# Reordering of inverse sums, weight units and first slot in a fused attention and two-layer kernel

## What is computed

```python
scores = cap * np.tanh(scale * np.matmul(q, k.transpose(0, 1, 3, 2)) / cap)
attn = np.exp(scores - np.max(scores, axis=-1, keepdims=True))
attn = attn / (np.sum(attn, axis=-1, keepdims=True) + 1e-09)
x = np.matmul(attn, v)                      # heads side by side: 896 x 768
h = x @ w_in                                # 768 -> 2048
x = np.where(h > 0.0, h, np.exp(np.minimum(h, 0.0)) - 1.0) @ w_out
h = x @ w_in2
return np.maximum(0.01 * h, h) @ w_out2
```

## Time and profile before

| | us |
|---|---|
| median of 3 runs (574.10 to 576.91) | 575.11 |
| the profiled execution's own time | 574.71 |
| its span | 572.9 |

### The profile page before, as it was taken

One profiled execution on the slowest core, in us unless ns is written; L12 is line 12 of the kernel. 1 busy time (PEld: TensorE's weight loads), 2 busy tenths in 40 slices (PEclk: granted clock), 3 DMA queues, 4 the chain that ended last, 5 costly groups with the idle time before them and its releaser, 6 DMA issues.

```text
span 572.9 us, 8610 instructions
## 1 busy us (share of the span) xinstructions
PE 556.7 (97%) x2908; PEld 499.4 (87%) x2908; DVE 469.4 (82%) x758; ACT 352.8 (62%) x606; POOL 275.2 (48%) x273
## 2 busy tenths in 40 slices
PE   6999989999999999999999999989999999999997
PEld 5777779889998999999999999879999998999997
DVE  5899998878875133898988999889999779999881
ACT  6999988999995455654644454536454445544440
POOL 6779998799965655552000003856666530000000
DMA  6455564455423333335644332031113225536251
GB/s 174 106 143 128 150 174 125 123 130 146 98 65 89 98 112 110 111 108 165 213 135 158 131 99 67 1 110 56 57 55 90 77 84 192 159 119 220 84 170 51
DMA packets 34172, 67.07 MB, mean 117 GB/s; under 512 B 6864, under 2 KB 18768, under 8 KB 34128
## 3 DMA queue, kind: packets, MB, share of 16 engines
q1 hardware_dynamic: 33984, 66.28, 39.4%
q10 hardware_dynamic: 144, 0.23, 0.1%
HBM read 63.70 MB, written 2.80 MB: 116 GB/s over the span
## 4 chain that ended last, share of the span: by engine, by line
PE 77%; DVE 10%; ACT 4%; issue 3%; POOL 3%; DMA 2%; ACTq 0%; SPq 0%; DVEq 0%; POOLq 0%
PE mlp_ps L1129 8%; PE mlp_ps L1131 8%; PE mlp_ps L1130 8%; PE o_ps L1129 6%; PE o_ps L1131 6%; PE o_ps L1130 6%; PE scores L1129 4%; PE scores L1130 4%; PE scores L1131 4%; PE probs_t L1103 4%; PE probs_t L1131 4%; PE probs_t L1130 4%; PE probs_t L1129 4%; PE scores L1088 2%; PE o_ps L1122 2%
## 5 line engine op out<-in xcount | busy, mean ns | idle before, releaser
L559 POOL TENSOR_TENSOR w_lo<-w_raw,w_hi 128x768 fp32r<-128x768 f32 (+1 forms) x62 | 104.2, 1681 | 62.3 <-ACT w_hi L621 61.9
L559 POOL TENSOR_TENSOR w_lo<-s_sum,w_hi 128x384 fp32r<-128x384 f32 x32 | 38.8, 1228 | 114.5 <-ACT w_hi L621 114.5
L621 ACT ACTIVATE w_hi<-s_sum 128x768 fp32r<-128x768 f32 (+1 forms) x64 | 43.4, 684 | 76.6 <-DVE s_sum L880 51.9
L621 ACT ACTIVATE w_hi<-w_raw 128x768 fp32r<-128x768 f32 (+1 forms) x77 | 56.5, 737 | 31.1 <-PE o_ps L1131 15.7
L601 ACT ACTIVATE soft<-soft,neg_max 112x448 f32<-112x448 f32 x96 | 63.6, 673 | 1.8 <-DVE soft L758 1.7
L758 DVE TENSOR_SCALAR_CACHE_REDUCE soft<-soft,neg_abs 112x448 f32<-112x448 f32 x96 | 60.9, 671 | 2.2 <-ACT soft L591 1.9
L1129 PE MATMUL mlp_ps<-x_hi,w_hi 128*128 128x448 f32 x132 | 49.2, 373 | 0.4 <-issue 0.4
L765 DVE TENSOR_TENSOR p_lo<-probs_t,p_hi 112x896 fp32r<-112x896 f32 x37 | 40.3, 1089 | 10.0 <-ACT p_hi L610 9.9
L1130 PE MATMUL mlp_ps<-x_lo,w_hi 128*128 128x448 f32 x132 | 48.2, 365 | 0.0
L1131 PE MATMUL mlp_ps<-x_hi,w_lo 128*128 128x448 f32 x132 | 48.2, 365 | 0.0
L591 ACT ACTIVATE soft<-scores 112x896 f32<-112x896 f32 x47 | 43.4, 924 | 6.0 <-PE scores L1089 5.9
(11 more groups left out here) (238 smaller groups left out, 1747.7 us busy)
## 6 DMA issues: line engine op xcount, KB each, us to landing
w_raw<-w_units SPq DMA_DIRECT2D x120, 384.0 KB, 3.2
q_raw<-qT SPq DMA_DIRECT2D x24, 224.0 KB, 3.1
k_raw<-kT SPq DMA_DIRECT2D x23, 224.0 KB, 3.0
v_raw<-v_rows SPq DMA_DIRECT2D x24, 112.0 KB, 3.2
inv_all<-inv_rows SPq DMA_DIRECT2D x24, 112.0 KB, 3.4
y_t<-y_out SPq DMA_DIRECT2D x12, 224.0 KB, 2.8
inv_rows<-row_inv SPq DMA_DIRECT2D x24, 1.8 KB, 3.1
k_raw<-kT ACTq DMA_DIRECT2D x1, 224.0 KB, 3.1
```

Source lines behind the costliest of these rows:

```text
L559: pool.tensor_tensor(w_part(w_lo, n), w_source(n), f32(w_part(w_hi, n)), ALU.subtract).then_inc(w_lo_pool, 1)
L621: nc.scalar.activation(w_part(w_hi, n), w_source(n), ACT.Copy).then_inc(w_hi_done, 1)
```

## The change

- SyncE: `store_inv` goes to the head of the odd step 2h+3, `load_inv` to the end of the even step 2h+4, behind the loads of k and q; loads of units go ahead of v.
- VectorE: `scale_o` goes from step 2h+7 to 2h+6, `w_high` of the first three units one step ahead. GpSimd: `x_parts` of the first four pairs go two steps ahead.
- Tables: step 30 has one chunk instead of three, step 54 ten instead of eight; a unit's last chunk is placed behind four chunks of the next unit, so that units end in every second step from 31 on.
- First slot: tanh and maxima tile by tile, the scale read from its column, the split of k of head 1 behind the maxima. All exponentials: each waits for its own tile's maximum.
- Border: the third `x_sum` comes ahead of a `weight_sum`, the last `weight_sum` of block 1 behind `y21`; in the first blocks the sums of (0, p6) and (0, p3) come ahead of `x_low("p2")`, and `block_hidden(0, "p3")` ahead of the sum of (0, p7).

```diff
@@ -2,2 +2,4 @@
+import itertools
+
 import numpy as np
@@ -47,3 +49,3 @@
 EARLY = {24: ((0, (0, 1, 2)),), 25: ((0, (3,)),), 26: ((1, (0, 1, 2)),), 27: ((1, (3,)),), 28: ((2, (0, 1, 2)),),
-         29: ((2, (3,)),), 30: ((0, (4,)), (1, (4,)), (2, (4,)))}
+         29: ((2, (3,)),), 30: ((0, (4,)),)}
@@ -56,3 +58,3 @@
          **{s: (1, 1, 0) for s in range(35, 48, 2)}, 48: (2, 1, 0), 49: (1, 2, 0), 50: (2, 1, 0), 51: (2, 0, 4),
-         52: (0, 0, 6), 53: (0, 0, 6), 54: (0, 0, 8)}
+         52: (0, 0, 6), 53: (0, 0, 6), 54: (0, 0, 10)}
@@ -64,3 +66,4 @@
-LATER = [(0, 5), (1, 5), (3, 0), (3, 1), (2, 5)] + [(u, c) for u in range(3, MAT_UNITS) for c in range(KC) if u > 3 or c > 1]
+LATER = [(0, 5), (1, 4), (1, 5), (3, 0), (2, 4), (3, 1), (3, 2), (3, 3), (2, 5), (3, 4)] + [
+    chunk for u in range(4, MAT_UNITS) for chunk in [(u, c) for c in range(4)] + [(u - 1, 5), (u, 4)]] + [(MAT_UNITS - 1, 5)]
@@ -74,6 +77,4 @@
     for n in MIXED.get(s, (0, 0, 0)):
-        place = {}
-        for u, c in LATER[done:done + n]:
-            place.setdefault(u, []).append(c)
-        places.append(list(place.items()))
+        runs = itertools.groupby(LATER[done:done + n], lambda chunk: chunk[0])
+        places.append([(u, [c for _, c in run]) for u, run in runs])
         done += n
@@ -162,3 +163,3 @@
 def x_step(m):
-    return 4 * m + (9 if 2 * m >= DIRECT else 11)
+    return 4 * m + 9
@@ -298,2 +299,3 @@
         y_stored = sem("y_stored")
+        first_scores, first_tanh = sem("first_scores"), sem("first_tanh")
         zero_set, ident_set, ident_ready = sem("zero_set"), sem("ident_set"), sem("ident_ready")
@@ -485,2 +487,9 @@
                     load_w(u + AHEAD + RAW)
+
+                if s % 2 == 1 and 0 <= (s - 3) // 2 < NHEAD:
+                    store_inv((s - 3) // 2)
+                if s in FIRST_LOADS:
+                    load_w(FIRST_LOADS.index(s))
+                if s % 2 == 1 and 2 <= s // 2 + 1 < NHEAD:
+                    load_v(s // 2 + 1)
                 if s % 2 == 0 and s // 2 + 4 < NHEAD:
@@ -488,10 +497,4 @@
                     load_q(s // 2 + 4)
-                if s % 2 == 1 and 0 <= (s - 5) // 2 < NHEAD:
-                    load_inv((s - 5) // 2)
-                if s % 2 == 1 and 2 <= s // 2 + 1 < NHEAD:
-                    load_v(s // 2 + 1)
                 if s % 2 == 0 and 0 <= (s - 4) // 2 < NHEAD:
-                    store_inv((s - 4) // 2)
-                if s in FIRST_LOADS:
-                    load_w(FIRST_LOADS.index(s))
+                    load_inv((s - 4) // 2)
             for r in range(units_ending_at(STEPS - 1)[0] + AHEAD + RAW, len(RAW_ROWS)):
@@ -587,2 +590,11 @@
             def tanh(k):
+                if k == 0:
+
+                    act.wait_ge(first_scores, 1)
+                    nc.scalar.activation(soft[0:QT, 0, 0, :], scores[0:QT, 0, 0:SEQ], ACT.Tanh, scale=s_scale[0:QT, 0:1]
+                                         ).then_inc(first_tanh, 1)
+                    act.wait_ge(scores_done, 1)
+                    nc.scalar.activation(soft[0:QT, 0, 1, :], scores[0:QT, 1, 0:SEQ], ACT.Tanh, scale=s_scale[0:QT, 0:1]
+                                         ).then_inc(tanh_done, 1)
+                    return
                 act.wait_ge(scores_done, k + 1)
@@ -596,3 +608,2 @@
                 b, c = k % SOFT, k % 2
-                act.wait_ge(neg_max_done, 2 * k + 2)
                 if half == 0 and h >= 2:
@@ -600,2 +611,3 @@
                 for t in range(2):
+                    act.wait_ge(neg_max_done, 2 * k + t + 1)
                     nc.scalar.activation(soft[0:QT, b, t, :], soft[0:QT, b, t, :], ACT.Exp, bias=neg_max[:, c, t:t + 1],
@@ -696,4 +708,5 @@
             act.wait_ge(cap_ready, 1)
-            act.reg_load(scale_reg, s_scale[0:1, 0:1].bitcast(mybir.dt.int32))
             for s in range(STEPS):
+                if s == 1:
+                    act.reg_load(scale_reg, s_scale[0:1, 0:1].bitcast(mybir.dt.int32))
                 if s < SLOTS:
@@ -755,4 +768,7 @@
                 b, c = k % SOFT, k % 2
-                dve.wait_ge(tanh_done, k + 1)
+                if k:
+                    dve.wait_ge(tanh_done, k + 1)
                 for t in range(2):
+                    if k == 0:
+                        dve.wait_ge(*((first_tanh, 1), (tanh_done, 1))[t])
                     nc.vector.tensor_scalar(soft[0:QT, b, t, :], soft[0:QT, b, t, :], neg_abs[0:QT, 0:1], BIG, ALU.mult,
@@ -981,3 +997,2 @@
             nc.vector.tensor_scalar(s_scale[:, :], cap_inv[:, :], float(HD) ** -0.5, None, ALU.mult).then_inc(cap_ready, 1)
-            split_k0(1)
             for s in range(STEPS):
@@ -985,2 +1000,4 @@
                     maxima(s)
+                if s == 0:
+                    split_k0(1)
                 for u in units_ending_at(s - 1):
@@ -991,6 +1008,6 @@
                     invert((s - 3) // 2)
-                if s in (12, 16, 20):
-                    w_high((s - 12) // 4)
-                if s % 2 == 1 and 0 <= (s - 7) // 2 < DIRECT:
-                    scale_o((s - 7) // 2)
+                if s in (11, 15, 19):
+                    w_high((s - 11) // 4)
+                if s % 2 == 0 and 0 <= (s - 6) // 2 < DIRECT:
+                    scale_o((s - 6) // 2)
                 if s % 2 == 0 and DIRECT <= (s - 6) // 2 < NHEAD:
@@ -1017,6 +1034,5 @@
             x_sum(y12, y12, y11, ALU.subtract)
+            x_sum(y11, y22, y11, ALU.add)
             weight_sum(GEMM1 + BLOCK_AT[1, "p3"])
             x_low("p5")
-            x_sum(y11, y22, y11, ALU.add)
-            weight_sum(GEMM1 + BLOCK_AT[1, "p7"])
             x_low("p6")
@@ -1024,2 +1040,3 @@
             add_to(0, "p4", y21, kept_u2[0], y21_done)
+            weight_sum(GEMM1 + BLOCK_AT[1, "p7"])
             for q in range(GEMM1 + 1, GEMM2[1] + 1):
@@ -1027,4 +1044,2 @@
                 i, p = BLOCK_SEQ[q - GEMM1 - 1]
-                if i == 0 and p == "p6":
-                    x_low("p2")
                 if p == "p6":
@@ -1033,4 +1048,5 @@
                     block_add(0, "p3")
-                    block_add(0, "p7")
+                    x_low("p2")
                     block_hidden(0, "p3")
+                    block_add(0, "p7")
                     block_hidden(0, "p7")
@@ -1089,2 +1105,4 @@
                     last = nc.tensor.matmul(dst[0:QT, t, 0:SEQ], q_stack[:, b, rows], k_lo[:, b, :], start=False, stop=True)
+                    if k == 0 and t == 0:
+                        last.then_inc(first_scores, 1)
                 last.then_inc(scores_done, 1)
```

2 lines of the change are left out of this document (1 added, 1 removed).

## The result

| | before | after |
|---|---|---|
| median, us | 574.61 (7 runs, 573.77 to 576.91) | 579.56 (7 runs, 577.75 to 581.11) |
| the profiled execution, us | 574.71 | 579.96 |
| its span, us | 572.9 | 578.2 |

The change makes the kernel slower: 1.0083 times, 95% interval 1.0068 to 1.0097, so 4.95 us. That is above my range (571.9 to 578.4) and in the class to which I gave 0.12.

A forecast was written before the change was run, and what follows sets the result against it. ScalarE, GpSimd and VectorE were taken to bound attention, TensorE the steps from 25 on. First slot 0, sums 0.2, units 0.3, step 54 0.9, border -0.5: 0.9 us lost, forecast 576.0 us, range 571.9 to 578.4.

The forecast's parts named there:

- I take 0, with ends of 0.3 us gain and 0.3 us loss: First slot: the wait for VectorE's second maximum goes, the later split of k delays slot 2; net 0.
- that very rule for the border: Border: VectorE with two SBUF inputs and GpSimd lock each other out, so long `x_low` and `x_sum` stay; 0.5 us gained.
- a loss of 0.2 us: Inverse sums and scaled O: last `p_low` ahead of step 25 ends at 80.8 instead of 80.66 us.
- the wait at head 5: VectorE's wait for the read-back of the inverse sums before scaled O: 1.3 us in place of 0.68.
- the rest is caught up by VectorE: Attention, steps 15 to 24: delay beyond ScalarE's gains is made up by VectorE, which had idled for late tanhs.
- Rival (c): Read-back behind the load of q lands later than 3.8 us; with 1.3 us more, 578.6 us; chance 0.13.
- Units and step 54: 0.3 and 0.9 us: Units: 0.9 us gained by step 37, 1.23 lost in step 54, sum 0.3 lost; wait for unit 15 0.9.
- I take 0.5 us gained: Border of the layers: VectorE's chain ends at about 382.5 instead of 383.05 us; ends 0 and 2.0.
- The last wait: Border: one TensorE wait of 1 to 1.6 us, behind VectorE's chain, in place of three.
- the chain now starts at the end of block (0, p6), 369.9 us: Border: VectorE's chain of sums, `x_low`, `x_sum` and p4 starts there, all parts as before, ending at about 382.5 us.
- The second goes: Border: TensorE's 1.4 us wait vanishes, `block_hidden(0, "p3")` being ready at about 374.8 for a bank wanted at 375.3 us.
- the first goes: Border: TensorE's 0.4 us wait ending at 368.28 us vanishes, since `x_sum` comes a `weight_sum` sooner.

The follow-up runs named there:

- the repair: The changed kernel with only SyncE's order changed, the read-back of the inverse sums issued ahead of the loads of k and q: 577.36 us, 1.0053.
- the line moved back: The changed kernel with the split of k of head 1 again ahead of the loop over steps: 578.04 us, 1.0053 of the kernel before.
- moved back beside the read-back: The changed kernel with the split of k of head 1 ahead of the loop and the read-back ahead of the loads: 575.20 us, 1.0005.

## Why the prediction was wrong

**First slot: "I take 0, with ends of 0.3 us gain and 0.3 us loss".** This is the step that failed most: 3.44 us in the profiled execution. I priced the moved split at its old 0.40 and 0.62 us. It was moved from a place where GpSimd is at its own first splits for only 0.2 us of it to one where GpSimd has 5 us of work without a pause, and there it took 1.7 to 3.4 us. I had also priced only ScalarE's delay; the gap in TensorE was 2.5 to 4.3 us instead of 1.84, and the clock fell in it in four of six profiles. The Trainium skill (SBUF — State Buffer, "SBUF: two separate sides") has VectorE and GpSimd take the shared pair of ports for a whole instruction, the other blocked meanwhile; the rows agree (0.62 us with GpSimd idle, 1.95 us beside its subtraction). I had used that very rule for the border and did not ask it of VectorE's subtraction here, which has two SBUF inputs as well. The copy has one, and stood too (0.81 to 1.45 us beside GpSimd's work against 0.40).

**Inverse sums: "a loss of 0.2 us".** Mis-sized: 1.3 us in the profiled execution, 1.6 alone. The place and the mechanism were right, and the wait at head 5 was met to 0.03 us. Two things failed: the wait at head 7 was 1.72 us and not 0.9, which goes with a read-back that took 4.0 us to land and not 3.4 to 3.8; and "the rest is caught up by VectorE" did not hold, since TensorE stood with it (1.68 us) and the clock was below full in the means of 76 to 80 and 80 to 84 us (0.74 and 0.83). Rival (c) had late landings behind the load of q, at 1.3 us for each of the two heads. At head 7 the landing took 4.0 us, above its 3.8, but at head 5, directly behind a load as well, 3.4, and the longest in the kernel, 5.1 us, is that of the last head; so (c) came about in a small part. What made head 7's landing long stays open. The median landing is 3.4 us behind the loads and 3.3 ahead of them, and single landings of 5.6 to 6.2 us are in the kernels with the read-back ahead too. The DMA engines' share doesn't explain it either: 0.98 from 57.0 to 60.5 us, during head 5's 3.4 us, and 0.82 from 69.5 to 73.7, during head 7's 4.0. What the repair does show is that an earlier read-back ends the waits: for head 5 it leaves at 51.08 us for a use at 57.38, and no longer at 57.04 for a use at 60.51. It moves the read-back to another time and to another place among the loads at once, and the two were not tried apart.

**Units and step 54: 0.3 and 0.9 us.** Right: 1.0 us gained by step 48 where I had 0.9, and 2.3 us in step 54 where I had 1.23 and 0.9; alone 1.6 us against 1.2.

**Border: "I take 0.5 us gained".** Wrong sign: 0.8 us lost in the profiled execution, 0.7 us in that of the part alone; by the medians 0.3 us, not told from 0. The last wait was right (1.38 us in the row). What failed is "the chain now starts at the end of block (0, p6), 369.9 us": VectorE's sum of weights now comes later, ScalarE stands 5.56 us for it, and its copy of (0, p1), next in its program, is made at 371.00 us instead of 368.10 (before the change); `block_add(0, "p6")` waits for that copy, starts at 371.63, and `x_sum` at 378.53 us instead of 377.60. This is read from the rows of the part alone; it was not tried by itself. "The second goes" failed too: `block_hidden(0, "p3")` was through at 376.2 us and not at 374.8, and TensorE's next wait, for the second of the two, was 0.33 us. So did "the first goes": the two `x_low` ahead of it now took 4.66 us together, where each took 1.56 before; VectorE in the kernel before, then in the part alone:

```profile
361.33 1.56 DVE L895 TENSOR_TENSOR p_lo<-y,p_hi 128x1344 fp32r<-128x1344 f32 x1
...
366.57 1.56 DVE L895 TENSOR_TENSOR p_lo<-y,p_hi 128x1344 fp32r<-128x1344 f32 x1
```

```profile
363.62 4.66 DVE L895 TENSOR_TENSOR p_lo<-y,p_hi 128x1344 fp32r<-128x1344 f32 x2
```

The long form of `x_low("p2")` and `x_sum` stayed (2.11 and 2.33 us), as the rule said.

**Sum.** With the measured sizes, 3.4 + 1.3 - 1.0 + 2.3 + 0.8 - 1.6 = 5.2 us. Of the miss of 3.6 us the first slot makes 3.4 in the profiled execution, and 1.7 to 2.8 by the medians (from 1.0083 to 1.0053 with the line moved back, from 1.0053 to 1.0005 with it moved back beside the read-back; alone in the kernel before it was 0.5); the sums make 1.1 to 1.4 and the border about 1, together more than the miss, since the pitch gave 1.6 back in the profiled pair. The range was too narrow since both ends of the first slot, 0.3 us to each side, rested on the split's old duration.

## What to carry to other kernels

Price a moved VectorE instruction by the rows of the place it goes to, not of the place it leaves: look what GpSimd does there, above all where the instruction reads two tiles of the SBUF. A small transfer that somebody waits for goes ahead of the big loads that nobody waits for yet, and ahead of any that must itself wait for a buffer. And when a change opens a gap in TensorE's work, count the gap twice: once as itself, and once for the clock that may fall in it.
